# The first head's q and k loaded and split in other pieces, and another order of output and gate steps around the last attention tile

## The reference, cut to what matters

```python
q, k, v: (2, 8, 1152, 64)
q_pool = q.reshape(B, H, S // 2, 2, D).mean(axis=3)          # 576 queries a head
scores = scale * np.matmul(q_pool, k.transpose(0, 1, 3, 2))  # 1152 keys
attn = exp(scores - max) / (sum + 1e-09)
attn_out = np.matmul(attn, v)
x = attn_out.transpose(0, 2, 1, 3).reshape(1152, 512)

x = (sigmoid(x @ w_gate) * (x @ w_val)) @ w_out              # d_ff 1536

P = exp(x @ w_gate2 - max); 8 x {rows, then columns normalised}
for e in range(8):
    out += P[:, e:e + 1] * (np.maximum(x @ w1[e], 0.0) @ w2[e])   # F = 1024
```

## Time and profile before

| | us |
|---|---|
| median of three runs | 1254.6 |
| the profiled execution, its own time | 1255.11 |
| its span in the trace | 1253.3 |
| TensorE busy | 1241.2 |
| VectorE busy | 748.9 |
| ScalarE busy | 584.5 |
| GpSimd busy | 574.2 |

### The profile page before, as it was taken

The page is one execution under the profiler, slowest core; times in us unless marked ns, Lnnn a source line. Parts: engine busy times, 40 slices in busy tenths (PEclk is TensorE's granted clock), DMA queues, the critical chain, the costliest instruction groups (busy, mean ns, idle before and its releaser), DMA issues.

```text
span 1253.3 us, 19795 instructions
## 1 busy us (share of the span) xinstructions
PE 1241.2 (99%) x7548; PEld 1139.9 (91%) x7548; DVE 748.9 (60%) x1618; ACT 584.5 (47%) x1233; POOL 574.2 (46%) x464
## 2 busy tenths in 40 slices
PE   8999999999999999999999999999999999999998
PEld 7888888999999899999999999999998998998997
DVE  6999999962223133867566466466466466466443
ACT  6999999943333234444353233233233233233221
POOL 5577777722122355745245255255255255255220
PEclk9999999999999999999999999999999999999999
DMA  7677676321110232122122122122122122122112
GB/s 171 109 120 118 123 121 122 78 61 51 33 50 26 84 96 73 40 79 85 45 77 81 40 82 81 46 79 79 49 77 77 51 77 75 54 79 71 52 35 93
DMA packets 98314, 95.29 MB, mean 76 GB/s; under 512 B 14449, under 2 KB 72305, under 8 KB 98225
## 3 DMA queue, kind: packets, MB, share of 16 engines
q1 hardware_dynamic: 97904, 93.51, 29.8%
q10 hardware_dynamic: 320, 0.59, 0.2%
HBM read 88.59 MB, written 2.40 MB: 73 GB/s over the span
## 4 chain that ended last, share of the span: by engine, by line
PE 93%; ACT 5%; DVE 1%; issue 1%; DMA 0%; POOL 0%; SPq 0%; DVEq 0%; POOLq 0%
PE bank L1028 12%; PE bank L1030 11%; PE bank L1029 11%; PE bank L1183 10%; PE bank L1182 10%; PE bank L1184 10%; PE bank L907 5%; PE bank L1005 4%; PE bank L1006 4%; PE bank L1007 4%; PE bank L882 4%; PE bank L920 3%; PE bank L921 3%; ACT probs L1276 2%; ACT pT_hi L1199 2%
## 5 line engine op out<-in xcount | busy, mean ns | idle before, releaser
L1669 DVE TENSOR_TENSOR c<-bank,c 128x256 f32<-128x256 f32 (+1 forms) x448 | 197.3, 456 | 280.3 <-PE bank L1030 268.1
L840 POOL TENSOR_TENSOR w_lo<-w_raw,w_hi 128x512 fp32r<-128x512 f32 x128 | 163.7, 1299 | 288.0 <-ACT w_hi L1199 288.0
L1183 PE MATMUL bank<-w_lo,h_hi 128*128 128x512 f32 x576 | 225.1, 391 | 0.0
L1182 PE MATMUL bank<-w_hi,h_hi 128*128 128x512 f32 x576 | 225.1, 391 | 0.0
L1184 PE MATMUL bank<-w_hi,h_lo 128*128 128x512 f32 x576 | 224.4, 390 | 0.0
L1394 ACT ACTIVATE h_hi<-c 128x256 fp32r<-128x256 f32 (+1 forms) x256 | 112.5, 445 | 160.1 <-DVE c L1669 159.8
L1184 PEld LDWEIGHTS bank<-w_hi,h_lo 128*128 128x128 f32 x576 | 108.2, 188 | 22.9
L1182 PEld LDWEIGHTS bank<-w_hi,h_hi 128*128 128x128 f32 x576 | 108.3, 188 | 20.8
L1183 PEld LDWEIGHTS bank<-w_lo,h_hi 128*128 128x128 f32 x576 | 108.3, 188 | 20.1
L1544 DVE TENSOR_REDUCE part_min<-bank 128x1 f32<-128x256 f32 (+2 forms) x216 | 114.6, 558 | 20.0 <-PE bank L921 13.3
L1199 ACT ACTIVATE c<-bank 128x256 f32<-128x256 f32 (+1 forms) x64 | 26.2, 410 | 214.6 <-PE bank L1030 214.6
(11 more groups left out here) (150 smaller groups left out, 2993.7 us busy)
## 6 DMA issues: line engine op xcount, KB each, us to landing
w_raw<-in_moe_w SPq DMA_DIRECT2D x64, 512.0 KB, 3.6
w_raw<-in_moe_w SPq DMA_DIRECT2D x64, 256.0 KB, 3.1
q_raw<-in_q SPq DMA_DIRECT2D x30, 288.0 KB, 6.2
k_raw<-in_k SPq DMA_DIRECT2D x30, 288.0 KB, 7.6
wo_raw<-in_moe_w_out SPq DMA_DIRECT2D x16, 384.0 KB, 3.5
v_raw<-in_v SPq DMA_DIRECT2D x16, 288.0 KB, 5.8
gv_raw<-in_moe_w_gate SPq DMA_DIRECT2D x12, 256.0 KB, 2.9
gv_raw<-in_moe_w_val SPq DMA_DIRECT2D x12, 256.0 KB, 3.2
```

Source lines behind the costliest of these rows:

```text
L840: ins = nc.gpsimd.tensor_tensor(w2_lo[:, u % 2, c], w2_raw[:, c], f32(w2_hi[:, u % 2, c]), ALU.subtract)
L1182: nc.tensor.matmul(bank[:, 3 + i], hh, wh, start=first, stop=False)
L1183: nc.tensor.matmul(bank[:, 3 + i], hh, wl, start=False, stop=False)
L1669: nc.vector.tensor_tensor(dst[:, 0:w], bank[:, (u + b) % 3, 0:w], other[:, 0:w], ALU.add).then_inc(done, 1)
```

## The change

For the first head, q is loaded as 128 and then 448 columns (`Q_BEGIN` from 256 to 128), and k as 256, 384 and 512 columns (`FIRST_KPIECES`). The last piece of k moves from ScalarE's DMA queue to SyncE's, between the two pieces of q. VectorE splits k in three pieces; the first scores wait for the first piece alone. GpSimd sums the 448 columns of q only when VectorE has split all of k. ScalarE rounds them ahead of the first exponential, not behind it, and VectorE takes their rest in tile 0, not in tile 1. For the second head GpSimd takes the rest of q ahead of the rest of k, not behind it.

In the last pair the steps of head 14 are those of the other pairs (9, 9, 9, 9, 6, 6, 6, 9, 9). ScalarE copies both halves of the partitions of head 14's first output, one tile later, and VectorE adds them in tile 8 instead of 6. Behind the last tile stand 18 steps of head 15, then the 9 transposes, `spread_recip`, the gate half of block (0,0) of the gated unit, and the other 18 steps. The warm-up has 28 transposes.

```diff
-AV_STEPS_LAST = (9, 9, 9, 9, 9, 9, 0, 9, 9)
-WARM_UP, WARM_TILE = 36, 9
-Q_BEGIN = 2 * PARTS
+WARM_UP, WARM_TILE = 28, 9
+Q_BEGIN = PARTS
+FIRST_KPIECES = ((0, 256), (256, 640), (640, 1152))
...
 # SyncE
+            load_first_q(slice(0, Q_BEGIN), q_begin_loaded)
+            k0, k1 = FIRST_KPIECES[2]
+            for half in range(2):
+                sp.dma_start(k_raw[0][rows_of(half), k0:k1], k_dram[0][:, k0:k1]).then_inc(k_loaded[0], 16)
+            load_first_q(slice(Q_BEGIN, QLEN), q_loaded[0])
             load_q(1)
...
 # GpSimd
-                split_k(h + 1)
-                pool.wait_ge(*k_there(h + 1, 2))
-                q_lo_part(h + 1)
+                    split_k(h + 1)
+                    pool.wait_ge(*k_there(h + 1, 2))
+                    q_lo_part(h + 1)
+                else:
+                    pool.wait_ge(q_summed[1], 1)
+                    q_lo_part(1)
+                    split_k(1)
...
             pool.wait_ge(q_loaded[0], 32)
+            pool.wait_ge(*k_there(0, 2))
             nc.gpsimd.tensor_tensor(q_sum[0][:, rest], ...)
...
 # TensorE
+                    elif h == LAST and u == 1:
+                        pe.wait_ge(tail_shifted, 1)
...
+                        pe.wait_ge(k_lo_done[0], 1)
...
-            for n in range(4 * KCH):
-                if n == 4:
-                    ... fill_p(g - 1, 0), fill_p(g - 1, 1)
-                if n == KCH:
-                    ... fill_p(g - 1, 2), spread_recip(0, 1)
-                av(NHEAD - 1, n)
+            for n in range(2 * KCH):
+                av(NHEAD - 1, n)
+            for j in range(NKB):
+                pe.wait_ge(exp_done, 2 * g - (1 if j < 2 else 0))
+                pe.wait_ge(p_lo_done, 3 * g - 5 + j)
+                fill_p(g - 1, j)
+            pe.wait_ge(r_done, NHEAD - 1)
+            spread_recip(0, 1)
+            pe.wait_ge(x_done, HEADS // 2)
+            pe.wait_ge(gv_split, 1)
+            f1_part(0, 0, 0, None)
+            for n in range(2 * KCH, 4 * KCH):
+                av(NHEAD - 1, n)
             pe.wait_ge(r_done, NHEAD)
             pe.wait_ge(p_lo_done, 3 * g)
             spread_recip(1, 4)
...
 # ScalarE
-                if i == 0 and pair == 0:
-                    q_hi_part(0)
-                if i == (6 if h < LAST else 5):
+                if i == 6:
                     o_out(h, 0, 0)
+                    if h == LAST and u == 0:
+                        copy(o_all[h % ORING][rows_of(a), cols], bank[rows_of(a), 7, 0:QHALF])
...
-            k_hi_part(0, 0)
-            k_hi_part(0, 1)
+            for piece in range(3):
+                k_hi_part(0, piece)
+            q_hi_part(0)
...
 # VectorE
-                if g == 1:
+                if g == 0:
                     dve.wait_ge(q_hi_done, 1)
                     first_q_lo(slice(Q_BEGIN, QLEN), q_lo_done[0])
-                if h == NHEAD - 1 and i == 6:
+                if h == NHEAD - 1 and i == 8:
                     add_rows(LAST, 0, 0)
```

More of the change, by code:

```diff
@@ L242, in build @@
         q_loaded = [sem(f"q_loaded{a}") for a in range(2)]
-        k_begin_loaded = sem("k_begin_loaded")
+        k_begin_loaded = [sem(f"k_begin_loaded{n}") for n in range(2)]
+        k_first_hi_done = sem("k_first_hi_done")
         q_begin_loaded = sem("q_begin_loaded")
@@ L397, in k_of @@
         def k_of(h, piece):
-            k0, k1 = KPIECES[piece]
+            k0, k1 = (KPIECES if h else FIRST_KPIECES)[piece]
             return k_st[h % KRING][:, k0:k1], k_raw[h % 2][:, k0:k1]
@@ L409, in k_there @@
         def k_there(h, pieces):
-            return k_lo_done[h > 0], 2 * (h - 1) + pieces if h else pieces
+            return k_lo_done[h > 0], 2 * (h - 1) + pieces if h else 1 + pieces
         def all_tiles(tile):
@@ L937, in tile @@
                 score(pair, i, 0)
+                if g == 0:
+                    pe.wait_ge(*k_there(0, 1))
                 score(pair, i, 1)
@@ L949, in tile @@
                         fill_p(g - 1, j)
-                steps = AV_STEPS_LAST if pair == NHEAD // 2 - 1 else AV_STEPS
                 if i < COMMON and pair >= 1:
-                    for n in range(sum(steps[:i]), sum(steps[:i + 1])):
+                    for n in range(sum(AV_STEPS[:i]), sum(AV_STEPS[:i + 1])):
                         av(2 * pair - 1, n)
@@ L956, in tile @@
                 if i >= COMMON:
-                    for n in range(sum(steps[COMMON:i]), sum(steps[COMMON:i + 1])):
+                    for n in range(sum(AV_STEPS[COMMON:i]), sum(AV_STEPS[COMMON:i + 1])):
                         av(2 * pair, n)
@@ L975, in spread_recip, with f1_part, f1_step @@
                 mm.then_inc(r_spread, 1)
[L977 to L989 removed]
+            def f1_part(a, blk, gv, freed):
+                if freed is not None:
+                    pe.wait_ge((sig_done, h32_done)[gv], freed)
+                dst = bank[:, 3 * gv + blk, 0:BLK].rearrange("p (a n) -> p a n", a=2)
+                for c in range(DCH):
+                    wh, wl = gv_hi[a][:, gv, c], gv_lo[a][:, gv, c]
+                    xh, xl = x1_block(x_hi, c, blk), x1_block(x_lo, c, blk)
+                    nc.tensor.matmul(dst, wh, xh, start=(c == 0), stop=False)
+                    nc.tensor.matmul(dst, wh, xl, start=False, stop=False)
+                    mm = nc.tensor.matmul(dst, wl, xh, start=False, stop=(c == DCH - 1))
+                mm.then_inc((g_ready, v_ready)[gv], 1)
+            def f1_step(a, blk, freed):
+                for gv in range(2):
+                    f1_part(a, blk, gv, freed)
+            g = PAIR * NHEAD // 2
+            for n in range(2 * KCH):
[10 more added lines that the diff above has]
+            for n in range(2 * KCH, 4 * KCH):
                 av(NHEAD - 1, n)
@@ L1017, in f1_first @@
                         pe.wait_ge(x_tail, NHEAD - LAST)
-                    f1_step(f, blk, FIRST_F1.index((0, blk)) + 1 if f else None)
+                    if n == 0:
+                        f1_part(0, 0, 1, None)
+                    else:
+                        f1_step(f, blk, FIRST_F1.index((0, blk)) + 1 if f else None)
             def f1(f, half, a):
@@ L1213, in k_hi_part @@
             def k_hi_part(h, piece):
-                if h == 0 and piece == 0:
-                    act.wait_ge(k_begin_loaded, 32)
+                if h == 0 and piece < 2:
+                    act.wait_ge(k_begin_loaded[piece], 32)
                 else:
                     act.wait_ge(k_loaded[h % 2], 32 * (h // 2) + 32)
-                nc.scalar.activation(*k_of(h, piece), ACT.Copy, scale=split_scale[:, 0:1]).then_inc(k_hi_done, 1)
+                nc.scalar.activation(*k_of(h, piece), ACT.Copy,
+                                     scale=split_scale[:, 0:1]).then_inc(k_hi_done if h else k_first_hi_done, 1)
             def p_hi(g, j):
@@ L1292, in gv_hi_part @@
                 copy(gv_hi[a][:], gv_raw[a][:]).then_inc(gv_hi_done, 1)
-            for piece, done in enumerate((k_begin_loaded, k_loaded[0])):
-                k0, k1 = KPIECES[piece]
+            for piece, done in enumerate(k_begin_loaded):
+                k0, k1 = FIRST_KPIECES[piece]
                 for half in range(2):
@@ L1506, in add_rows @@
                 dve.wait_ge(tail_shifted, 2 * (h - LAST) + u + 1)
-                nc.vector.tensor_tensor(o_all[h % ORING][rows_of(a), cols], bank[rows_of(a), o_bank(h, u), 0:QHALF],
-                                        tail_other(a)[:, cols], ALU.add).then_inc(o_copied, 1)
+                own = o_all[h % ORING][rows_of(a), cols]
+                part = own if h == LAST and u == 0 else bank[rows_of(a), o_bank(h, u), 0:QHALF]
+                nc.vector.tensor_tensor(own, part, tail_other(a)[:, cols], ALU.add).then_inc(o_copied, 1)
             def finish_tail(h, a):
@@ L1577, in _ @@
             first_q_lo(first, q_begin_lo_done)
-            split_first_k(0)
-            split_first_k(1)
+            for piece in range(3):
+                split_first_k(piece)
             all_tiles(tile)
```

31 lines of the change are left out of this document (5 added, 26 removed).

## The result

The change won 2.07 us where 3.0 were forecast. The kernel after took 1253.05 us (median of 22 runs, 1252.20 to 1254.37), the kernel before 1255.12 (22 runs, 1254.13 to 1256.15); the ratio is 0.9985, 95% interval [0.9978, 0.9991]. That is within the 0.2% that the prediction called no change. The time lies at the upper end of the range given (1253.2). Of the 1.45 us between it and the 1251.6 forecast, 0.5 is the base: the three runs shown of before had their median at 1254.6.

The account below looks back on a forecast made before the run. TensorE, busy 1241.2 of 1253.3 us, was taken to bound the kernel. Terms 1.6 (tile 1) + 1.2 (tile 4) + 0 (last pair) + 0.2 (behind the last tile) = 3.0, so 1254.6 - 3.0 = 1251.6 us, range 1250.4 to 1253.2.

Parts of the forecast that it names:

- tile 4: TensorE's 1.2 us wait for GpSimd's `q_lo` ahead of tile 4 goes, v's split still in time: 1.2 us won.
- the last pair: Steps of the last two heads only spread otherwise: 0 counted, bounds 0.4 us lost to 0.2 won.
- tile 1: Second exponential at 13.9 instead of 15.52, held by the second head's q: 1.6 us won.
- behind the last tile: Two groups of transposes become one, saving a wait and a switch: 0.2 us won, bounds 0 and 0.4.
- Tile 0: First exponential at 10.3 instead of 12.22, set by the other 448 q columns, expected to land at 8.5.
- this landing hardly moves: Second head's q, landed at 10.82 before, lands at 11.0 (bounds 10.4 and 11.9), since the bytes ahead are the same.
- the data is late: Rival: smaller pieces and issue gaps delay q at the start; total 2.0 us won, 1252.6; chance 0.20.
- My sentence on bandwidth: Start's DMA: the skill measures 138 GB/s for 64 KB transfers, 341 for 1 MB; the change makes 64 KB pieces.
- the k split: VectorE's split of k beside GpSimd's sum took 1349 ns, against 816 for more columns; lock rule said not to change the sum.
- the prediction's own signs: Prediction is wrong if, among others, a later stage gives the 3 us back by a wait absent in the trace before.
- The clock: Rival: start's idle stretches drop the clock to 1.2 GHz, three tiles 2.7 us longer each: 1259.6; chance 0.04.
- what is won at the start is won at the end: Behind the start every stage is TensorE's, so gains there were to reach the end in full.

Follow-up runs that it names:

- e1: Kernel before with only the change's loads, splits and orders of the first two heads; 1254.96 us, ratio 0.9991 to before.
- e4: Changed kernel with head 14's first add moved from tile 8 to behind the splits of the last transposes; 1254.73 us, ratio 0.9984 to before.
- e5: Changed kernel with GpSimd's split of the second gate block waiting for VectorE's add of tile 8; one execution, 1254.28 us.
- e6: Changed kernel with ScalarE's rounding of the second head's q behind tile 0's two copies, not ahead; one execution, 1253.27 us.
- e9: Changed kernel once more, unaltered; 1253.01 us, ratio 0.9980 to before.
- e10: Changed kernel with the late add, the same edit as e4, on another chip; 1253.16 us, ratio 0.9982 to before.
- e12: Changed kernel with 21 dummy transposes in tile 0 instead of 9; 1254.43 us, ratio 0.9993 to before.
- e13: Changed kernel without the 9 dummy transposes in tile 0; 1252.98 us, ratio 0.9983 to before.
- e15: Changed kernel again, unaltered, on a fourth chip; 1253.12 us, ratio 0.9983 to before.
- e2: Kernel before with only the change's last-pair steps, moved add and stream behind the last tile; 1256.89 us, ratio 1.0002 to before.
- e3: Kernel before with one edit: GpSimd takes the second head's rest of q ahead of the rest of k; 1256.49 us, ratio 0.9996 to before.
- e7: Changed kernel with the first 640 columns of k in one DMA per half of the partitions; one execution, 1254.44 us.
- e11: Changed kernel with the late add of e4 and the single k transfer of e7; 1252.40 us, ratio 0.9976 to before.
- e14: e11 with 18 dummy transposes in tile 0 instead of 9; 1253.02 us, ratio 0.9981 to before.
- e8: Changed kernel with e4's late add, e6's rounding, and GpSimd's second sum behind VectorE's rest of the first q; 1255.19 us, ratio 0.9982 to before.

## Why the prediction was wrong

Two terms of the sum held, at tile 4 and in the last pair; the terms at tile 1 and behind the last tile were mis-sized. The profile's own sum is 1.04 + 1.23 - 0.13 - 0.56 = 1.58 (the 0.13 is what the lead lost from tile 4 to tile 71).

*Tile 0.* Forecast 10.3, came 10.62: 448 columns landed at 8.88, not 8.5. It didn't matter, as said.

*Tile 1: the term was 1.6 and measured 1.04.* The step that failed is "this landing hardly moves". With the change's transfers GpSimd's second sum started at 11.70 in the profile of after and from 10.94 to 11.48 in nine others (e1, e4, e5, e6, e9, e10, e12, e13, e15; mean of the ten 11.28). With before's it was 10.82, 10.85 and 10.87 (before, e2, e3), and with k in one transfer 11.19, 10.90 and 10.69 (e7, e11, e14; mean 10.93). (e8 is left out, since its sum waits for VectorE.) So the smaller pieces cost some 0.4 us by these means, most of which one transfer of k gives back, and 11.70 came late by chance.

Single landings overlap (11.19 in e7), but two other numbers do not: the traffic from 2 to 4 us was 168 to 193 GB/s with the change's transfers in all eleven traces, 230 to 249 with before's, 233 to 235 with k in one transfer; and the 448 columns of the first head landed at 8.21 to 8.32 with k in one transfer, at 8.61 to 9.14 with the small pieces (e1 left out, where GpSimd waits for VectorE). The second head's q is also issued 1.3 us later than before (4.87 against 3.57), but so it is in e7, e11 and e14, so that is not what costs the most. Tile 1 followed 2.77 or 2.78 us behind the sum in after and in e4, e5, e7, e11, e12, e13 and e14 (full clock, rounding in the change's place): late data goes through in full. (The chain behind the sum is 2.78, not the 2.90 of my sum, and the first head has 1.18 MB, not 1.15; neither matters.)

This is the rival "the data is late", to which I had given 0.20. Its total, 2.0, is close to the 2.07 measured, but in part by luck: it foresaw neither the held add nor the losses in the middle of the attention. By the mean landing, 11.28, tile 1 comes at 14.06 and the term is 1.46, near the forecast; the late landing in this profile made it 1.04. My sentence on bandwidth was the better guide: the Trainium skill (DMA: Bandwidth & Descriptors, "Bandwidth") has small transfers at a lower rate. The trace agrees in direction, 172 GB/s against 249; the page's figures are of transfers issued from GpSimd, and these are issued from SyncE and ScalarE.

*Tile 4: 1.2 forecast, 1.23 won,* with the v split ended at 24.69 against 24.1 forecast. It fits.

*The last pair: 0 forecast.* The lead of 2.24 us at tile 69 is 2.15 at tile 70: 0.09 lost, within the bounds.

*Behind the last tile: 0.2 forecast to be won, 0.56 lost* in the profile of after. The failed step is the price of the moved add, which I didn't give at all: I counted that a second copy was added on ScalarE and treated the add as the same instruction at a later place. Its operands had changed. So one of the prediction's own signs came: a later stage gives time back by a wait that the trace of before doesn't have, TensorE's for `pT_lo`. Where the add is not held, or is held but ends early enough, the tail is 27.10 to 27.14 (e4 to e8 and e10 to e15), 0.14 to 0.18 below before, as forecast. The price is the time that GpSimd's instruction has left, and it decides from some point on:

| | add ends behind GpSimd's instruction | add ends behind tile 71's exponential | tail |
|---|---|---|---|
| e15 | 0.31 | 1.24 | 27.13 |
| e9 | 0.31 | 2.64 | 27.63 |
| after | 0.31 | 2.86 | 27.84 |
| e2 | 0.30 | 3.04 | 28.04 |

Up to 1.79 us behind the exponential (e7, 1.32 us long, tail 27.12) the end costs nothing, and beyond 2.14 it costs all: 2.86 - 2.14 = 0.72 in after, whose tail is 0.71 above 27.13. The 2.14 is read back from the tails of e9, after and e2, which give 2.13 to 2.15. Where `gv_lo` stands hangs on the landing of v and of the other half's output, so I take it that the loss comes in part of the executions: of the seven profiles with the add in the change's place and GpSimd's stream unaltered (after, e6, e7, e9, e12, e13, e15) two have it. The Trainium skill (SBUF — State Buffer, "SBUF: two separate sides") has the rule: VectorE with two SBUF inputs and GpSimd exclude each other for a whole instruction, and the traces agree, with the 0.30 or 0.31 us behind GpSimd's end. I had held it against the k split, where it changed nothing, and not against the instruction whose operands the diff moved from PSUM to SBUF.

*The clock.* I gave a fall 0.04 and a price of 8 us: three tiles at twice TensorE's time. It came in 10 of 44 executions, and cost 1.3: the medians with and without it are 1254.14 and 1252.85, and in e9, e10 and e15 tile 2 came 1.29, 1.43 and 1.27 behind sum + 2.78 + 3.30. The price is small because it lasted 3.4 us, not three tiles. The mean clock is below full in 11 of 110 executions of before too, but 8 of these stand among the 50 on the two chips with the losses in the middle. On the other two it is 3 of 60, against 5 of 22 of the changed kernel there, which points to more falls with the change. That idle time is the cause is not shown: 2.06 (e5), 2.17 (e1) and 2.76 us (e13) left the clock full, and 1.79, 2.05 and 2.10 did not. In e11 (1.28 us idle) and e14 (0.20) it never came.

*What is missing in the medians.* Of the 3.0 forecast 0.93 did not come. An estimate from the traces: the falls 0.2 (1253.07 with them, 1252.85 without); the landing 0.15 (1.46 at tile 1 instead of 1.6); the last part 0.2 (the mean tail of the seven profiles named above is 27.30, level with before, where 0.2 was to be won). The rest, some 0.4, would lie between tile 4 and tile 71, where I forecast no loss: measured against the one profile of before, the lead shrank there by 0.13 in after, 0.28 in e9 and 0.64 in e15, and by 1.95 in e12 and 1.48 in e14. So "what is won at the start is won at the end" did not hold in full either; the cause of these losses is open, and none of the shares is measured by itself.

## What to carry to other kernels

When an edit moves an operand from PSUM to SBUF, price the instruction anew: beside a GpSimd instruction on SBUF the add here lasted until that one had ended. Where a chain hangs on the landing of data, look at what smaller first transfers leave idle in the DMA engines: here 0.16 MB less in two microseconds came back as a landing some 0.4 us later. Making the early piece small on one queue only and keeping the others whole (e11) did best, in one comparison. And one profile of a kernel isn't its median: three of the same kernel differed by 1.0 us here, by a landing, a held add and a fall of the clock.

## What the hardware showed that I had not expected

- An add with both inputs in SBUF ended 0.30 or 0.31 us behind the GpSimd instruction beside it, in eight profiles (after, e2, e5, e6, e7, e9, e13, e15; 0.44 us became 0.78 to 2.58). With one input in PSUM it was not held (0.44 us in e1 beside GpSimd's `v_st`), nor were three `pT_lo` in after, 1.48 us at 252.09 beside GpSimd's multiply of 251.48 to 252.90.
- The landing of one transfer varied by 0.8 us (10.94 to 11.70) between profiles with the same transfers ahead of it.
- The granted clock was half for 3.4 us, from 12.5 to 13 us on, in three profiles (e9, e10, e15) and full in others of the same kernels (after, e4).
- ScalarE stood still for 1.8 us ahead of a copy in e12 with nothing that a view shows as late.
